# The rounding of the gated hidden tile and its low part placed straight behind the gate on ScalarE and VectorE

## The reference

```python
out_d = sm_attn(mean4(q), mean4(k), mean4(v))        # softmax attention on means of 4 positions
out_local = softmax(scale*q@k.T, |i-j| < 4) @ v      # band of 7 keys
x = tokens(repeat4(out_d) + out_local)               # 2304 x 512
h = x @ w_in                                         # 512 -> 2048
g = h * clip(h + 3, 0, 6) / 6                        # the gate
x = g @ w_out                                        # 2048 -> 512
h = max(x @ w1, x @ w2, x @ w3)                      # 512 -> 768
out = h @ moe2_w_out                                 # 768 -> 512
```

## Time and profile before

| | |
|---|---|
| time, median of 3 runs | 841.81 us (841.18 to 846.93) |
| the profiled execution | 841.3 us, of which the profile's span is 839.5 us |
| busy over the span | PE 813.3 us (97%), DVE 343.6 us (41%), ACT 291.4 us (35%), POOL 146.1 us (17%) |
| TensorE's granted clock | 0.99 of full speed in the mean |
| steps 0 to 79 | 57 us to about 540 us; attention in them until about 375 us |

### The profile page before, as it was taken

How to read it: one execution, slowest core, us unless ns; L and a number is a source line. 1 busy time by engine, 2 the same in 40 slices (tenths; PEclk the granted TensorE clock), 3 DMA queues, 4 the chain that set the end, 5 groups by cost and what they waited for, 6 DMA issues and landing times.

```text
span 839.5 us, 12737 instructions
## 1 busy us (share of the span) xinstructions
PE 813.3 (97%) x5372; PEld 694.0 (83%) x5372; DVE 343.6 (41%) x611; ACT 291.4 (35%) x618; POOL 146.1 (17%) x107
## 2 busy tenths in 40 slices
PE   7778998999999999999999999999999999999998
PEld 6556877888888888888998999888888888888897
DVE  4957777656445564443333222233113112202211
ACT  5545645454343443433232344221112111111111
POOL 4733545410122110210000144200000000000000
PEclk8899999999999999999999999999999999999999
DMA  8852621122211222102000433200020020020010
GB/s 164 200 180 79 159 59 45 40 79 59 60 33 49 83 59 59 31 1 96 1 1 0 132 115 112 85 0 1 26 75 1 13 88 0 1 76 0 13 39 26
DMA packets 93477, 49.06 MB, mean 58 GB/s; under 512 B 61164, under 2 KB 86252, under 8 KB 93420
## 3 DMA queue, kind: packets, MB, share of 16 engines
q1 hardware_dynamic: 90740, 47.36, 20.2%
q10 hardware_dynamic: 2680, 0.89, 0.5%
HBM read 38.79 MB, written 9.44 MB: 57 GB/s over the span
## 4 chain that ended last, share of the span: by engine, by line
PE 85%; DVE 9%; ACT 4%; issue 1%; DMA 1%; SPq 0%; DVEq 0%; ACTq 0%
PE bank L650 27%; PE bank L652 26%; PE bank L651 26%; DVE gs L1300 3%; PE bank L771 1%; PE bank L748 1%; DVE lp_a L1210 1%; ACT w L1003 1%; PE bank L697 1%; DMA q_nat_b<-in_q_dram 1%; PE bank L723 1%; PE bank L710 1%; ACT dp_a L964 1%; DVE lp_a L1195 1%; PE bank L737 1%
## 5 line engine op out<-in xcount | busy, mean ns | idle before, releaser
L650 PE MATMUL bank<-xs,w 128*128 128x512 f32 (+3 forms) x680 | 255.2, 375 | 2.0 <-DVE rg L1293 1.5
L651 PE MATMUL bank<-xs,w 128*128 128x512 f32 (+3 forms) x680 | 252.2, 371 | 0.0
L652 PE MATMUL bank<-xs,w 128*128 128x512 f32 (+3 forms) x680 | 252.2, 371 | 0.0
L650 PEld LDWEIGHTS bank<-xs,w 128*128 128x128 f32 x680 | 127.9, 188 | 22.7 <-issue 2.8
L652 PEld LDWEIGHTS bank<-xs,w 128*128 128x128 f32 x680 | 127.9, 188 | 19.3
L651 PEld LDWEIGHTS bank<-xs,w 128*128 128x128 f32 x680 | 128.0, 188 | 18.5
L650 PE MATMUL bank<-gs,w 128*128 128x460 f32 (+1 forms) x320 | 122.0, 381 | 6.6 <-DVE gs L1300 6.6
L1293 DVE SCALAR_TENSOR_TENSOR rg<-rg,bank 128x460 f32<-128x460 f32 (+1 forms) x80 | 50.7, 633 | 174.5 <-ACT rg L1030 174.3
L652 PE MATMUL bank<-gs,w 128*128 128x460 f32 (+1 forms) x320 | 118.8, 371 | 0.0
L651 PE MATMUL bank<-gs,w 128*128 128x460 f32 (+1 forms) x320 | 118.6, 371 | 0.0
L1030 ACT ACTIVATE rg<-bank,half 128x460 f32<-128x460 f32 (+1 forms) x80 | 51.7, 646 | 186.4 <-PE bank L652 174.2
(11 more groups left out here) (200 smaller groups left out, 869.2 us busy)
## 6 DMA issues: line engine op xcount, KB each, us to landing
w_raw<-in_moe_w_out_dram SPq DMA_DIRECT2D x22, 256.0 KB, 4.3
w_raw<-in_moe_w_dram SPq DMA_DIRECT2D x18, 256.0 KB, 3.0
out_dram<-o_sb SPq DMA_DIRECT2D x18, 256.0 KB, 2.0
w_raw<-in_moe_w_in_dram SPq DMA_DIRECT2D x16, 256.0 KB, 3.7
xr<-x_scratch SPq DMA_DIRECT2D x4, 1024.0 KB, 6.3
q_nat_a<-in_q_dram SPq DMA_DIRECT2D x26, 144.0 KB, 3.0
v_a<-in_v_dram SPq DMA_DIRECT2D x24, 144.0 KB
k_nat_a<-in_k_dram SPq DMA_DIRECT2D x24, 144.0 KB, 3.0
```

What stands on the lines that cost most here:

```text
L650: mm(dst, w[0], m[0], start=start, stop=False, skip_group_check=True)
L651: mm(dst, w[0], m[1], start=False, stop=False, skip_group_check=True)
L652: return mm(dst, w[1], m[0], start=False, stop=stop, skip_group_check=True)
```

## The change

In each step, ScalarE does `gate_high(s + 1)` straight behind `gate_relu(s + 1)`, ahead of slot 2s and of the weight rounding `high_w1(s + 3)`. VectorE does `gate_low(s + 1)` straight behind `gate(s + 1)`, ahead of slot 2s. TensorE, GpSimd and SyncE keep their order. No instruction is added or taken away.

```diff
@@ scalar
                 if s + 1 < STEPS:
                     gate_relu(s + 1)
+                if s + 1 < STEPS:
+                    gate_high(s + 1)
                 attend(2 * s)
                 if s + 3 < F1:
                     high_w1(s + 3)
-                if s + 1 < STEPS:
-                    gate_high(s + 1)
                 attend(2 * s + 1)
@@ vector
                 if s + 1 < STEPS:
                     gate(s + 1)
-                attend(2 * s)
                 if s + 1 < STEPS:
                     gate_low(s + 1)
+                attend(2 * s)
                 attend(2 * s + 1)
```

## The result

The changed kernel takes 852.5 us in the median (4 runs, 850.56 to 854.88) beside 842.43 us for the kernel before (841.18 to 846.93). The ratio is 1.0105, with a 95% interval of 1.0073 to 1.0136: slower by 8.9 us by the ratio and by 10.1 by the medians. The profiled execution has a span of 848.8 us where that of before had 839.5, 9.3 more.

What follows compares the result with a forecast made beforehand. TensorE was taken as the bound, fully busy from 171 to 376 us. Terms of 8.0 + 1.2 + 0.7 = 9.9 us on the profiled 841.3 gave 851.2, and 0.5 for the median made 851.7 us; range 846 to 855.

Steps and rivals of the forecast that it cites:

- The delay: ScalarE in even slots behind a gate: the slot's work starts 1.31 us later than before.
- Term 1: Starts of pairs 8 to 15: TensorE's scores wait for later copies on ScalarE, 8.0 us in all.
- Term 2: Ends of pairs 11 and 15: the split of x comes late for the next chunk's hidden tile, 1.2 us for both.
- Term 3: First 13 steps: waits for the low part go, others replace them; steps from 171 us on start about 0.7 us later.
- The walk for pair 4: First steps, engine by engine: late copies, split, mask, weights and divisions make the next hidden tile about 1.3 us later.
- the low part's mean at 460 columns: Sign on VectorE, line 1300: the mean should fall towards 0.7 us.
- the early gain stays: Rival, first steps: the 6.3 us of low-part waits go, only copies of pairs 4 and 6 replace them; 846.5 us, chance 0.14.
- the copies are half covered: Rival, pairs 8 to 15: half the copies' delay does not reach TensorE; 847 us, chance 0.08.
- the first steps lose 4 us or more: Rival, first steps: VectorE and GpSimd lock, each even pair loses 2 to 3 us more; 855 or more, chance 0.13.
- Behind the steps: Behind 376 us, no attention in the steps: same work at the same time, 0 us.

Runs made afterwards that it cites:

- a1: Kernel before with only ScalarE's rounding moved straight behind gate_relu, VectorE's low part left in place: 850.26 us, ratio 1.0093.
- a2: Kernel before with both parts of the change in steps 15 to 79 only: 849.59 us, ratio 1.0074.
- a4: Kernel before with the change in all steps but ten (starts of pairs 8 to 15, steps 30 and 46): 845.48 us, ratio 1.0024.
- b1: Changed kernel with one more, unread rounding ahead of the copies where pairs 8 to 15 begin: 857.9 us, ratio 1.0161 to the kernel before.
- a3: Kernel before with both parts of the change in steps 0 to 14 only: 843.08 us, ratio 1.0005.
- c1: a3 with GpSimd's low_w1 moved behind slot 2s + 1: 840.45 us, ratio 0.9977 to the kernel before.
- c3: Kernel before with only GpSimd's low_w1 moved behind slot 2s + 1: 838.96 us, ratio 0.9952.
- b4: Kernel before with ScalarE's rounding ahead of high_w1 and GpSimd's low_w1 behind slot 2s + 1: 838.05 us, ratio 0.9924.
- c2: Same kernel as b4, timed again in more rounds against the kernel before: 837.96 us, ratio 0.9936.
- b3: Kernel before with ScalarE's rounding moved ahead of high_w1, still behind slot 2s: 842.21 us, ratio 0.9981.

## Why the prediction was right

Predicted were 851.7 us and measured are 852.5. That the two lie within 0.8 us is in part luck, since the kernel before came out at 842.4 beside this run and not at 841.8. What compares like with like is the trace: 9.9 us were expected, and 9.0 are found in the two stretches that the change touches (1.3 and 7.7). Part of that agreement is luck too: the first two terms were 1.3 and 0.3 us too large, the third 0.6 too small.

**The delay.** Predicted 1.31 us between the old and the new start of the slot's work on ScalarE, measured 1.30 (1.85 less 0.55).

**Term 1, pairs 8 to 15.** Predicted 8.0 us, measured 6.7, as the growth of the lag of the scores' starts over the eight pairs (0.80, 0.98, 0.71, 0.75, 0.88, 1.10, 0.76 and 0.75). The mechanism was right and the handover was mis-sized: I took 0.14 us from pair 13, whose scores started that long behind the copy, for the time from a copy's end to the scores. With TensorE waiting it is 0.05 us, so pair 13 had 0.09 us of slack and each pair costs 0.09 less. The copies also run a little shorter than before, 177.44 being 2.32 us after the start of the first one where it was 2.36. These two make 1.0 of the 1.3 us. a1, a2, a4 and b1 show the term from four sides: where it is made (ScalarE), in which steps, in which ten of them, and that it grows one for one.

**Term 2, the split ahead of a chunk.** Predicted 0.6 us twice, measured 0.57 and 0.36. VectorE at pair 11, which answers to the earlier trace rows, and TensorE behind it:

```profile
273.61 0.64 DVE L1293 SCALAR_TENSOR_TENSOR rg<-rg,bank 128x462 f32<-128x462 f32 x1 [3.44 <-ACT rg L1030]
274.90 0.64 DVE L1300 TENSOR_TENSOR gs<-rg,gs 128x462 fp32r<-128x462 f32 x1 [0.66 <-ACT gs L1038]
275.46 1.17 DVE L1256 TENSOR_TENSOR x<-bank,down_a 128x232 f32<-128x232 f32 x4
277.09 0.40 DVE L1265 TENSOR_TENSOR xs<-x,xs 128x232 fp32r<-128x232 f32 x1 [0.46 <-ACT xs L998]
...
277.54 0.48 PE L650 MATMUL bank<-xs,w 128*128 128x462 f32 x1 [0.43 <-DVE xs L1265]
```

From the gate's start to `put_x` it is 1.85 us where it was 0.91, 0.94 more as predicted. Pair 15 had more slack than pair 11, which I had set equal: in the kernel before, its split ended 0.60 us ahead of the hidden tile and pair 11's 0.39.

**Term 3, the first steps.** Predicted 0.7 us later, measured 1.3 in the trace and 0.4 in a3's ratio, whose interval goes from -1.6 to +2.4 us. The walk for pair 4 held in its order: the split under the weights, the mask at 72.20 (predicted 72.05), the weights at 80.35 (80.1), the divisions done at 83.97 and 85.42 (84.1 and 85.3), the next hidden tile at 85.98. The last two times agree by luck. The first division took 1.29 us and not the 1.65 of the earlier trace rows, and the second did not follow it at once, as I had taken it, but waited 0.31 us for VectorE's inverse, which I had not in the walk. At pair 6 two errors cancel: the waits for GpSimd are 2.2 us where I had 1.2, and the wait of 0.8 for the mask, which the walk does not name, went. Summed from the waits, pair 4 costs 0.9 us (predicted 1.3), pair 6 wins 0.6 (0.7), and pairs 5 and 7 cost 0.2 and 0.6, which I had near nothing. I had not foreseen the 0.5 us for the load of k at pair 7. As forecast, the low part's mean at 460 columns fell, to 654 ns over all 48 of that form, and that of the splits rose, at 116 columns from 409 to 802 ns:

```profile
L1300 DVE TENSOR_TENSOR gs<-rg,gs 128x460 fp32r<-128x460 f32 x48 | 31.4, 654 | 31.5 <-ACT gs L1038 31.5
...
L1265 DVE TENSOR_TENSOR xs<-x,xs 128x116 fp32r<-128x116 f32 x8 | 6.4, 802 | 3.3 <-ACT xs L998 3.3
```

(from the groups by form, with busy time, mean ns of one, and idle time before them).

**The rivals.** That the early gain stays is excluded by a3, and c1 shows whose order made the waits that took its place. That the copies are half covered is excluded by the eight waits. That the first steps lose 4 us or more is excluded by stretch A, which lost 1.3. What a3 and c1 leave open is how the remaining 1 us of the first steps divides: the waits for the gate (1293), the load and the mask are each under 1 us, and none was tried by itself.

**Behind the steps** with attention nothing moved, as predicted.

## What to carry to other kernels

An engine that is idle two thirds of the time can still set the pace of the bound one: look at the gap between the end of its work and the use of it, at the place where the instruction is to be put, and pay for the wait that comes with it as well as for its duration. Here a rounding of 0.5 us brought 0.7 us of waiting for another engine with it, in a place where six pairs had about 0.5 us to spare and two had 0.1 to 0.2.

Before moving a late instruction forward, ask what makes it late. Here it stood under another engine's long instruction, and moving that one (GpSimd's weights) gave what moving the late one did not.

## What the runs showed that I had not expected

The VectorE instructions with both inputs in SBUF that I looked at paid the whole rest of GpSimd's, the short ones too: a split of 0.27 us took 2.40 under GpSimd's 2.40, and in c3 a low part that started at 80.76 took 4.70 us, over two of GpSimd's in a row (80.23 to 84.97). One with a single input did so as well, line 1238 with its 1.22 us in place of 0.15. Whether a slow one costs anything depends on who waits for it: in c3 no matmul waited for that low part, while line 1238 held GpSimd's second division.

TensorE's granted clock fell in some executions for some microseconds in the first steps, behind a stretch with waits, and in others with the same order not. a3 and a4 have the same order up to step 14 and the same waits. Their stretches 80 to 90 and 90 to 100 us (PE, PEld, DVE, ACT, POOL busy, then the granted clock), a3's first:

```profile
80.00:90.00 10.00, 6.92 (x80) 5.46 (x80) 5.38 (x6) 4.40 (x10) 7.17 (x4) 1.00 0.00 0
90.00:100.00 10.00, 9.95 (x96) 8.39 (x92) 5.88 (x13) 6.69 (x11) 4.86 (x4) 1.00 0.68 176
```

and a4's, with one more of its stretches, 140 to 150:

```profile
80.00:90.00 10.00, 6.93 (x33) 5.78 (x32) 4.83 (x5) 4.46 (x9) 7.13 (x4) 0.79 0.00 0
90.00:100.00 10.00, 10.00 (x90) 8.18 (x88) 4.08 (x9) 5.14 (x9) 2.71 (x2) 0.87 0.37 90
...
140.00:150.00 10.00, 9.12 (x84) 7.58 (x81) 2.87 (x7) 4.07 (x9) 2.19 (x2) 0.83 0.22 50
```

Ahead of both, TensorE was busy 9.17 of 10 us from 70 to 80. a4 took 120.5 us for stretch A and a3 116.0. Means of 0.79, 0.87 and 0.83 over ten microseconds each fit a part of them at the lower of the two levels, 1.2 GHz: 2.1, 1.3 and 1.7 us lost, 5.1 in all, against the 4.5 by which a4's stretch is the longer. That is nearly as much as the runs of one kernel differ by (841.04 to 847.21 in a3). The ten runs of the kernel with both moves (b4 and c2), in whose steps no wait is longer than 1.5 us, all lie between 837.3 and 839.5. But b3, which has no longer one either, spreads from 839.38 to 844.78, so the length of the longest wait is not what decides it, and the reason for the narrower spread stays open.
